# A three-stage MLP chain on one core: second products of layer 2 in pairs on TensorE, layer 2 eleven units behind

## What is computed

```python
x = causal_conv(x, softmax(weight))        # 7 taps, 8192 tokens x 192
h = x @ w_in                               # 192 -> 2048
P = a[0] + a[1]*h + a[2]*h*h + a[3]*h*h*h
Q = 1.0 + abs(b[0])*abs(h) + abs(b[1])*h*h
x = (P / (Q + 1e-6)) @ w_out               # 2048 -> 192
h = x @ w_in2                              # layer 2
out = (s * max(h, 0)**2 + b2) @ w_out2     # 2048 -> 192
```

## Time and profile before

| | us |
|---|---|
| median of 3 runs (lowest to highest) | 1335.89 (1335.84 to 1336.78) |
| the profiled execution's own time | 1336.83 |
| its span, from the first to the last instruction | 1335.0 |
| busy in the span: PE / DVE / ACT / POOL | 1259.8 / 1160.5 / 1098.3 / 333.9 |
| mean granted TensorE clock | 0.982 of full speed |

### The profile page before, as it was taken

The page is one execution under the profiler, slowest core; times in us unless marked ns, Lnnn a source line. Parts: engine busy times, 40 slices in busy tenths (PEclk is TensorE's granted clock), DMA queues, the critical chain, the costliest instruction groups (busy, mean ns, idle before and its releaser), DMA issues.

```text
span 1335.0 us, 16225 instructions
## 1 busy us (share of the span) xinstructions
PE 1259.8 (94%) x5920; PEld 1069.3 (80%) x5920; DVE 1160.5 (87%) x1073; ACT 1098.3 (82%) x1053; POOL 333.9 (25%) x145
## 2 busy tenths in 40 slices
PE   3665899999999999999999999999999999999998
PEld 2544688888888888888888888888888888888887
DVE  7999999998899989999899989999899998978810
ACT  4766788888888888888888888888898888888833
POOL 4233222222222222222222222222222222222200
PEclk9787899999999999999999999999999999999999
DMA  5310100001000100001000010001000000000000
GB/s 134 103 32 0 24 1 12 1 1 36 0 12 0 36 0 0 12 0 36 0 12 0 0 36 0 12 0 36 0 0 12 0 12 1 13 1 13 0 13 12
DMA packets 17885, 20.40 MB, mean 15 GB/s; under 512 B 1472, under 2 KB 13760, under 8 KB 17600
## 3 DMA queue, kind: packets, MB, share of 16 engines
q1 hardware_dynamic: 17712, 20.00, 5.5%
q10 hardware_dynamic: 144, 0.01, 0.0%
HBM read 13.72 MB, written 6.29 MB: 15 GB/s over the span
## 4 chain that ended last, share of the span: by engine, by line
PE 75%; DVE 12%; ACT 6%; issue 5%; POOL 0%; DVEq 0%; ACTq 0%
PE o L340 22%; PE h L314 7%; PE h L317 7%; PE h L315 7%; PE h L316 7%; PE h L318 7%; PE o_tail L329 3%; PE o L327 3%; PE o L328 3%; PE o_tail L331 3%; PE o L330 3%; DVE work L610 3%; DVE work L651 2%; DVE work L649 1%; DVE work L612 1%
## 5 line engine op out<-in xcount | busy, mean ns | idle before, releaser
L297 POOL TENSOR_TENSOR gl<-work,gh 128x1024 fp32r<-128x1024 f32 x128 | 309.1, 2415 | 913.2 <-ACT gh L477 913.2
L340 PE MATMUL o<-v,work 128*128 128x192 f32 x2048 | 355.8, 327 | 3.4 <-ACT work L492 3.4
L340 PEld LDWEIGHTS o<-v,work 128*128 128x128 f32 x2048 | 338.2, 190 | 20.9 <-ACT work L492 11.2
L314 PE MATMUL h<-x_hi,w_hi 128*128 128x512 f32 x512 | 226.5, 442 | 61.5 <-DVE work L615 40.6
L610 DVE SCALAR_TENSOR_TENSOR work<-work,coef,h 128x1024 f32<-128x1024 f32 x128 | 163.6, 1278 | 91.9 <-ACT work L470 91.9
L317 PE MATMUL h<-x_tail,w_tail_hi 128*128 128x512 f32 x512 | 206.6, 403 | 0.0
L315 PE MATMUL h<-x_lo,w_hi 128*128 128x512 f32 x512 | 206.3, 403 | 0.0
L468 ACT ACTIVATE work<-h,coef 128x1024 f32<-128x1024 f32 x128 | 153.9, 1203 | 63.2 <-PE h L318 58.1
L316 PE MATMUL h<-x_hi,w_lo 128*128 128x512 f32 x512 | 205.8, 402 | 0.0
L318 PE MATMUL h<-x_tail,w_tail_lo 128*128 128x512 f32 x512 | 204.6, 400 | 0.0
L480 ACT ACTIVATE work<-work 128x1024 f32<-128x1024 f32 x128 | 135.9, 1062 | 65.7 <-DVE work L610 63.9
(11 more groups left out here) (62 smaller groups left out, 1563.2 us busy)
## 6 DMA issues: line engine op xcount, KB each, us to landing
out_dram<-y_out SPq DMA_DIRECT2D x16, 384.0 KB, 2.6
xt<-in_x_main_dram SPq DMA_DIRECT2D x7, 518.0 KB, 4.7
xt_tail<-in_x_tail_dram SPq DMA_DIRECT2D x8, 259.0 KB, 5.4
work<-in_moe_w_out_dram SPq DMA_DIRECT2D x1, 1536.0 KB, 10.9
v<-in_moe_w_out_dram SPq DMA_DIRECT2D x1, 1536.0 KB, 7.2
work<-in_moe_w_in_dram SPq DMA_DIRECT2D x1, 1024.0 KB, 9.3
work<-in_moe_w_in_dram SPq DMA_DIRECT2D x2, 512.0 KB, 5.6
xt<-in_x_main_dram SPq DMA_DIRECT2D x2, 259.0 KB, 4.9
```

The source lines that it names most:

```text
L297: nc.gpsimd.tensor_tensor(gl[:, j % 2, :], r_buf[j % 2], gh[:, j % 2, :].bitcast(F32), ALU.subtract).then_inc(gl_ready, 1)
L314: pe.matmul(h[:, half, :], hi[:, c], x_hi[:, :], start=True, stop=False)
L340: last = pe.matmul(o2[:, c // 2, c % 2, 0:D], g, v2[:, f, :], start=(f == 0 and c % 2 == 0), stop=(f == FT - 1), skip_group_check=True)
```

## The change

`SKEW` goes from 12 to 11. TensorE's order is written for two steps at a time. An even step is now F1(n), S1(n-3), S2(n-12), S2(n-11); an odd one is F1(n), F2(n-11), S1(n-3), F2(n-10). After the end of layer 1 the second products go one by one again. ScalarE's order alternates too: in an even step L489 and L492 of layer 2 come first and the copy to gh (L477) keeps its place behind L470; in an odd step the copy to gh comes first, ahead of L468, and L489 and L492 follow L470. On VectorE the whole split of o1 moves to step j = 2, between L615 and L649, where it was in three parts at j = 3; y_out moves from step 4 to the start of step 3; two tail taps and, in the first pass, some pair taps change their step. ScalarE's copy L463 moves from the start of step 3 to behind L470 in step 2.

```diff
-    SKEW = 12
...
+    SKEW = 11
     OUT1_LAG = 3
-    OUT2_LAG = 1
-    X2_STEP = OUT1_LAG
...
-    TAPS_AT = {(0, 1): (("pair", 0), ("tail", 0)), (0, 2): (("pair", 1),), (0, 4): (("tail", 1),),
+    X2_STEP = OUT1_LAG - 1
...
+    TAPS_AT = {(0, 1): (("pair", 0), ("tail", 0)), (0, 3): (("tail", 1),), (0, 4): (("pair", 1),),
                (0, 5): (("pair", 2),), (0, 6): (("pair", 3), ("tail", 2)), (0, 7): (("pair", 4),),
-               (1, 0): (("pair", 5), ("tail", 3)), (1, 1): (("pair", 6), ("tail", 4)),
-               (1, 2): (("tail", 5), ("tail", 6))}
+               (1, 0): (("pair", 5), ("tail", 3)), (1, 1): (("pair", 6),), (1, 3): (("tail", 4),),
+               (1, 4): (("tail", 5), ("tail", 6))}
...
-    SPLIT_A, SPLIT_A_FIRST = (1, 5), (1, 6)
...
+    SPLIT_A, SPLIT_A_FIRST = (1, 5), (1, 7)
...
-                two_buffers = isinstance(n, int) and n <= SKEW
+                two_buffers = isinstance(n, int) and n < SKEW
...
+            def first_of_layer_2(m, j, t, parity):
+                if unit(m):
+                    k = (j - SKEW) % UNITS
+                    back = (j - SKEW) // UNITS
...
+                    pe.wait_ge(u_ready, counted(m))
+                    x2p = (parity + back) % 2
+                    first_product(h2, k, w2_hi, w2_lo, w2_tail_hi, w2_tail_lo,
+                                  x2_hi[x2p], x2_lo[x2p], x2_tail[x2p], h2_ready)
...
+            def second_of_layer_2(m, j, t):
+                if unit(m):
+                    k = (j - SKEW) % UNITS
...
+                    pe.wait_ge(g2_ready, counted(m + 1))
+                    second_product_2(k, (j - SKEW) % 2)
+            def second_of_layer_1(n, j, t):
+                if unit(n - OUT1_LAG):
...
+                    pe.wait_ge(gh_ready, counted(n - OUT1_LAG + 1))
+                    pe.wait_ge(gl_ready, counted(n - OUT1_LAG + 1))
+                    second_product_1(k, (j - OUT1_LAG) % 2)
...
                 for j in range(UNITS):
-                    n, m = n0 + j, n0 + (j - SKEW)
...
+                    n = n0 + j
...
-                    if tile(t):
-                        second_product_of_layer_2(t, j, m, k2)
...
-                    if unit(m):
...
-                        pe.wait_ge(u_ready, counted(m))
...
-                    if not tile(t):
-                        second_product_of_layer_2(t, j, m, k2)
-                    if unit(n - OUT1_LAG):
...
+                    merged = tile(t) or n <= LAST_MERGED
+                    if j % 2 == 0:
+                        second_of_layer_1(n, j, t)
+                        second_of_layer_2(n - SKEW - 1, j - 1, t)
+                        if merged or n + 1 - SKEW == NU:
+                            second_of_layer_2(n - SKEW, j, t)
+                    else:
+                        first_of_layer_2(n - SKEW, j, t, parity)
+                        second_of_layer_1(n, j, t)
+                        if not merged and n - 1 > LAST_MERGED and unit(n - SKEW):
+                            second_of_layer_2(n - SKEW - 1, j - 1, t)
+                        first_of_layer_2(n - SKEW + 1, j + 1, t, parity)
...
+            def high_of_g(n, buf):
+                if unit(n - 2):
+                    act.wait_ge(g_ready, counted(n - 1))
+                    act.wait_ge(out1_done, counted(n - 3))
+                    nc.scalar.copy(gh[:, buf, :], r_buf[buf]).then_inc(gh_ready, 1)
+            def layer_2(m, buf):
+                if unit(m):
+                    act.wait_ge(h2_ready, counted(m + 1))
+                    act.wait_ge(g2_ready, counted(m))
+                    nc.scalar.activation(u_relu, h2_flat, ACT.Relu).then_inc(u_ready, 1)
+                    act.wait_ge(u_ready, counted(m + 1))
+                    act.wait_ge(out2_done, counted(m - 1))
+                    nc.scalar.activation(g2[1 - buf], u_relu, ACT.Square).then_inc(g2_ready, 1)
...
             def phase(n0, t, i, parity):
...
-                    if j == X2_STEP and tile(t - 1):
-                        act.wait_ge(out1_done, counted(t * UNITS))
-                        act.wait_ge(x2_tail_lo_ready, counted(t - 1))
-                        nc.scalar.copy(x2_sum, o1_tail[TAIL:P, :]).then_inc(x2_tmp_ready, 1)
+                    if j % 2 == 0:
+                        layer_2(m, buf)
+                    else:
+                        high_of_g(n, buf)
                     h_flat = h2_flat if in_h2(n) else h1_flat
...
-                    if unit(n - 2):
-                        act.wait_ge(g_ready, counted(n - 1))
-                        act.wait_ge(out1_done, counted(n - 3))
-                        nc.scalar.copy(gh[:, buf, :], r_buf[buf]).then_inc(gh_ready, 1)
+                    if j == X2_STEP and tile(t - 1):
+                        act.wait_ge(out1_done, counted(t * UNITS))
+                        act.wait_ge(x2_tail_lo_ready, counted(t - 1))
+                        nc.scalar.copy(x2_sum, o1_tail[TAIL:P, :]).then_inc(x2_tmp_ready, 1)
+                    if j % 2 == 0:
+                        high_of_g(n, buf)
+                    else:
+                        layer_2(m, buf)
...
-                    if unit(m):
-                        act.wait_ge(h2_ready, counted(m + 1))
...
-                        act.wait_ge(out2_done, counted(m - 1))
-                        nc.scalar.activation(g2[buf], u_relu, ACT.Square).then_inc(g2_ready, 1)
...
-                    if j == X2_STEP and tile(t - 1) and not second(t):
-                        split_o1(t, hi, lo)
-                        sum_o1_tail(t)
+                    if j == Y_STEP and tile(t - 2):
+                        dve.wait_ge(out2_done, counted((t - 1) * UNITS))
+                        dve.wait_ge(y_stored, counted((t - 2) * 16))
+                        for half in range(2):
...
-                    if j == (SKEW + OUT2_LAG + UNITS - 1) % UNITS and tile(t - 2):
...
-                    if j == X2_STEP - 1 and second(t):
...
+                    if j == X2_STEP and tile(t - 1):
                         split_o1(t, hi, lo)
                         sum_o1_tail(t)
                         split_o1_tail(t, tail)
...
-                    if j == X2_STEP and tile(t - 1) and not second(t):
-                        split_o1_tail(t, tail)
```

More of the change, by code:

```diff
@@ L57, in conv_rational_relu2_kernel @@
                      (1, 0): (("pair", 2), ("tail", 2)), (1, 1): (("pair", 3), ("tail", 3)),
-                     (1, 3): (("pair", 4), ("tail", 4)), (1, 4): (("pair", 5), ("tail", 5)),
-                     (1, 5): (("pair", 6), ("tail", 6))}
-    SPLIT_A, SPLIT_A_FIRST = (1, 5), (1, 6)
+                     (1, 3): (("tail", 4),), (1, 4): (("pair", 4), ("tail", 5)), (1, 5): (("pair", 5),),
+                     (1, 6): (("pair", 6), ("tail", 6))}
+    SPLIT_A, SPLIT_A_FIRST = (1, 5), (1, 7)
     SPLIT_B, SPLIT_B_FIRST = (0, 0), (0, 5)
@@ L359, in product_of_layer_1 @@
                               x1_hi[parity], x1_lo[parity], x1_tail[parity], h1_ready)
-            def second_product_of_layer_2(t, j, m, k2):
-                if unit(m - OUT2_LAG):
-                    k = (k2 - OUT2_LAG) % UNITS
+            def first_of_layer_2(m, j, t, parity):
+                if unit(m):
+                    k = (j - SKEW) % UNITS
+                    back = (j - SKEW) // UNITS
                     if k == 0:
-                        tk = t + (j - SKEW - OUT2_LAG) // UNITS
-                        pe.wait_ge(y_ready_out, counted(tk * 2))
+                        for ready in (x2_hi_ready, x2_lo_ready, x2_tail_hi_ready, x2_tail_lo_ready):
+                            pe.wait_ge(ready, counted(t + back + 1))
+                        pe.wait_ge(w_hi_ready, 10)
+                        pe.wait_ge(w_lo_ready, 12)
+                    pe.wait_ge(u_ready, counted(m))
+                    x2p = (parity + back) % 2
+                    first_product(h2, k, w2_hi, w2_lo, w2_tail_hi, w2_tail_lo,
+                                  x2_hi[x2p], x2_lo[x2p], x2_tail[x2p], h2_ready)
@@ L369, in second_product_of_layer_2 @@
+            def second_of_layer_2(m, j, t):
+                if unit(m):
+                    k = (j - SKEW) % UNITS
+                    if k == 0:
+                        pe.wait_ge(y_ready_out, counted((t + (j - SKEW) // UNITS) * 2))
                         pe.wait_ge(bias_row_ready, 1)
                         pe.wait_ge(v2_loaded, 16)
-                    pe.wait_ge(g2_ready, counted(m - OUT2_LAG + 1))
-                    second_product_2(k, (j - OUT2_LAG) % 2)
+                    pe.wait_ge(g2_ready, counted(m + 1))
+                    second_product_2(k, (j - SKEW) % 2)
@@ new lines, in second_of_layer_1 @@
+            def second_of_layer_1(n, j, t):
+                if unit(n - OUT1_LAG):
+                    k = (j - OUT1_LAG) % UNITS
+                    if k == 0:
+                        pe.wait_ge(x2_lo_ready, counted(t))
+                        pe.wait_ge(x2_sum_ready, counted(t))
+                        if first(t):
```

(15 more changed lines are left out.)

31 lines of the change are left out of this document (6 added, 25 removed).

## The result

| | before | after |
|---|---|---|
| median of the runs (lowest to highest), us | 1335.87 (1335.76 to 1336.78) | 1507.10 (1505.07 to 1507.26) |
| span of the profiled execution, us | 1335.0 | 1505.2 |
| mean granted TensorE clock | 0.982 | 0.949 |

The changed kernel takes 1.1277 times as long as the one before, 95% interval 1.1257 to 1.1296. The forecast was 1496 us with a range of 1460 to 1540.

A forecast was written before the change was run, and what follows sets the result against it. TensorE set the pace before; the early copy would make ScalarE's wait for VectorE's g the bound. 1335.0 + 20.4 (fill) + 133.2 + 15.7 (passes) - 8.8 (drain) = 1495.5, forecast 1496 us, range 1460 to 1540.

The forecast's parts named there:

- What bounds the kernel: Steady loop: TensorE sets the pace without gaps, VectorE and ScalarE near the limit, g hardly ready when the copy asks.
- The copy's waits for g: Sign in ScalarE's odd steps: the copy to gh waits for VectorE's L655, some 300 us in all.
- The even leg: Even L468 to odd L468: 10.85 us plus VectorE's extra work of even steps, 15.0 us per pass.
- The odd leg: Odd L468 to next even one: bound by ScalarE alone, running layer 2 twice, 9.4 us.
- the conv split at (1,5): VectorE's SPLIT_A in an odd step: 2.1 us against 1.9 us of room, adding 0.2 us per pass.
- The clock: Rival: TensorE's clock falls in odd-step waits, F2 takes 4.4 us; 13 to 45 us more, 1509 to 1541; chance 0.22.
- TensorE's busy share: Sign over the whole span: TensorE's busy share falls to near 84% (1252 of 1496).
- The fill: Start of the kernel: odd units 3 to 15 each idle VectorE 3.35 us, less 3.1 already idle: +20.4 us.
- The steady stage: Units 15 to 127, seven passes: six cost 22.2 us more each, 133.2, and the last 15.7.
- The drain: From the last L468 to the end: 72.4 us against 81.2, so -8.8 us with the shorter lag.
- What TensorE gains: Steady stage: two S2 in a row save one 0.14 us switch per two steps, 8 us over some 58 pairs.
- the rival of a faster kernel: Rival: TensorE stays the bound, saving 8 us of switches and up to 7 from shorter lag; about 1322 us; chance 0.05.

The follow-up runs named there:

- the last filled run: Changed kernel plus zero-weight filler matmuls on TensorE in the gaps of odd steps, none at (1,7): 1498.1 us, 1.121 times the kernel before.
- The last version: Against the kernel before: TensorE pairs, lag 13, copy to gh behind h1 reads, VectorE work re-placed, part of o1's split on ScalarE: 1326.4 us, ratio 0.993.

## Why the prediction was right, and where it was off

**What bounds the kernel, right.** The prediction read from the earlier trace rows that g was hardly ready when asked for 2.1 us behind the read of h1, and that a copy ahead of the read must wait. The copy's waits for g went from 4.4 to 254 us in the loop (302 in the whole span, some 300 said), and its place alone makes 124 us on the kernel before and takes 138 off the changed one.

**The even leg, right to 0.2%.** Eight times 10.85 plus 15.0 us of extra work is 101.8 us; measured 102.0. The lightest is 10.97 us (10.85 said), the one with the split of o1 14.14 (14.15 said). That the work of even steps lies on the path one to one was tested by moving 6.3 us of it: 6.5 came back.

**The odd leg, too small by 0.8 us in a pass.** Said were 75.4 us, measured 76.2, of which 0.9 disappear with the fillers (75.3). Its usual length was 9.35 us, 9.4 said, and the conv split at (1,5), for which 0.2 us were added, cost nothing (9.35).

**The clock, a rival that was half true.** Behind a wait of 2.65 us TensorE's matmuls started 0.43 us apart and the halves of the product 2.30 us, in place of 0.23 and 1.17:

```profile
751.14 0.80 PE L317 MATMUL h<-x_hi,w_hi 128*128 128x512 f32 x1 [2.65 <-ACT work L476]
751.73 0.63 PE L318 MATMUL h<-x_lo,w_hi 128*128 128x512 f32 x1
...
753.44 0.63 PE L317 MATMUL h<-x_hi,w_hi 128*128 128x512 f32 x1
...
755.09 0.39 PE L317 MATMUL h<-x_hi,w_hi 128*128 128x512 f32 x1
```

That is the lower level, 1.2 GHz, with the upper one, 2.4 GHz, back before the product's end at 755.1. The rival took the whole product at the lower level, 4.4 us, and 13 to 45 us for the kernel. The product took 3.95 us, the next F1 was at full speed, and h1 came only 0.3 us late in such a leg (757.62 - 747.97 = 9.65). There are 24 legs like it, two of 10.9 us and the first one, 12.8 us in all: 11.3 in the 26, and 1.5 in the first, whose F1 took 3.83 us in place of 2.35. That is the lower end of the rival's 13 to 45. With the gaps filled the kernel is 9.0 us faster, though 2.0 us are lost at the loop's start and the first leg keeps its low clock. So the rival and the forecast were both true in part: without the low clock the time is 1498 us by the last filled run and some 1494 by the legs, against 1496 said. It is also why TensorE's busy share fell to 88% and not to the 84% forecast. The rule of the Trainium skill that was cited ("TensorE: Matmul & The Clock Gate", Part 1), that the default state is throttled and activity releases it, agrees: with activity put in the gaps the granted clock stays at 1.00.

**The fill, 3.9 us too high, and what it hid.** Each odd unit made VectorE idle 3.3 us or more, as said. Summed up to its first operation of unit 15, VectorE's idle time grew by 22.2 us and not by 20.4: of the 3.1 us of waits that the prediction took off, 1.8 are still there, ahead of the operations at 154.44 and 176.44. Two things went the other way. The sum forgot that the change also moves the first conv split from (1,6) to (1,7) (`SPLIT_A_FIRST`), so 2.1 us of VectorE's work left the stretch before unit 15. And in the kernel before three operations of VectorE in this stretch started while GpSimd worked and took some 2 us longer than others of their kind, each ending 0.3 to 1.1 us behind GpSimd's end:

```profile
73.28 2.31 DVE L534 CAST x_hi<-conv 128x512 fp32r<-128x512 f32 x1
...
106.19 3.31 DVE L651 SCALAR_TENSOR_TENSOR work<-work 128x1024 f32<-128x1024 f32 x1
...
114.37 3.39 DVE L513 SCALAR_TENSOR_TENSOR conv<-xt,cw,conv 128x1024 f32<-128x1024 f32 x1
```

The changed kernel's shifted timing leaves one of these collisions, which takes 4.0 us off. The prediction had no term for them, so that part is luck. The split came back behind unit 15: the next F1 stands in line for it, and at the low clock,

```profile
195.04 0.79 PE L317 MATMUL h<-x_hi,w_hi 128*128 128x512 f32 x1 [1.57 <-DVE x_tail L563]
```

and the first odd leg took 12.29 us, 2.9 above the usual, 1.5 of it the clock and 1.4 the split. The step that was off is the list of VectorE's moved work: it had the table of the loop and not that of the first pass. In the run with the taps in odd steps the same wait was priced, at 1.6 us, and the clock behind it was not.

**The steady stage, 13.2 us too low in all.** 162.1 us were measured for units 15 to 127 and 148.9 worked out. The even legs sum to 707.5 us, 706.3 said: 1.2. The odd legs sum to 538.2, 527.6 said: 10.6, which is 11.3 of low clock and the 2.9 of the first leg, less 3.6 for usual legs that were 0.05 us shorter than said and the 0.2 of the conv split. And the sum took seven passes of 155.0 us for the kernel before, whose last pass is 153.6: 1.4. The fill's error covered some of this, so the forecast lies nearer to the result than its terms do.

**The drain, right.** 72.7 us, 72.4 said (the last read of h1 at 1432.50, the last operation of VectorE at 1501.06, 4.1 us before the end; in the earlier trace rows 1253.85 and 1330.85).

**What TensorE gains, wrong, though nothing of the forecast hung on it.** Two S2 in a row, then the first matmul of F1:

```profile
759.72 5.36 PE L343 MATMUL o<-v,work 128*128 128x192 f32 x32
764.78 0.53 PE L317 MATMUL h<-x_hi,w_hi 128*128 128x512 f32 x1
765.15 0.40 PE L318 MATMUL h<-x_lo,w_hi 128*128 128x512 f32 x1
```

They take 5.06 us to the start of F1, where twice 2.46 is 4.92, and the first matmul of F1 still takes 0.37 us. Apart, two S2 cost 2 x (2.46 + 0.14) = 5.20 us with their switches; in a row 5.06 + 0.14 = 5.20. So nothing is saved. The prediction took 0.14 us for the price of leaving the fp32 product, but the second S2 adds 2.60 us and not 2.46: an S2 is 2.60 us of work, and the product behind it starts before the last of it is over. The last version confirms it, for there TensorE is busy without a gap: two steps take 19.15 us, where 19.04 was worked out and 19.17 to 19.18 were taken before. The 8 us that the pairing was to give, and that the rival of a faster kernel counted on, are not there. In the changed kernel this lies in the even leg, in which TensorE is not the last, so the error does not show in its time.

## What to carry to other kernels

When an instruction with a wait moves ahead in an engine's order, lay out the loop it closes: from the engine, through the other engines, back to what it waits for, in starts and ends of one period; a wait of 4 us in total before says that the slack is used up, not that there is plenty. In a schedule of period two, work of a helper engine is free in one half and costs its full length in the other, so it is placed by the half, and tables for the first pass have to be read like those of the loop. The price of a switch between two kinds of work is to be read over both sides of it: what the second kind loses, the first may have gained. Where a helper's result is moved in time, look at what its work now runs beside: VectorE pays for some overlaps with GpSimd. A busy engine that begins to wait may lose clock as well; filling its gaps with harmless work shows what that costs, if the legs are read and not the time alone.
